# Products with v for halves of two neighbouring heads side by side, and one block-diagonal last product for both

## The reference

```python
B, H, S, D = 2, 8, 768, 64
mask = q_bucket[:, :, :, None] == k_bucket[:, :, None, :]
scores = np.where(mask, scale * q @ k.T, -1e9)
attn = np.exp(scores - scores.max(-1)); attn /= attn.sum(-1) + 1e-09
x = attn @ v                    # then [B*S, H*D]
logits = x @ w_gate             # 8 experts; the largest takes the token
eom = sigmoid(x @ w_output_gate)
out[token] = gate_w * eom * expert(x)     # then the dense pair
```

## Time and profile before

| | |
|---|---|
| median of 3 runs | 790.98 us |
| profiled execution | 790.95 us, span 789.1 us |
| granted TensorE clock, mean | 0.998 |
| TensorE busy | 775.8 us (98%), 4359 records |
| VectorE, ScalarE, GpSimd busy | 451.7, 376.7, 340.1 us |
| attention stage | up to about 263 us |
| records of `times_v` | 66.8 us busy in bank_b, 372 records |
| records of `last` | 23.5 us busy, 192 records |

### The profile page before, as it was taken

How to read it: one execution, slowest core, us unless ns; L and a number is a source line. 1 busy time by engine, 2 the same in 40 slices (tenths; PEclk the granted TensorE clock), 3 DMA queues, 4 the chain that set the end, 5 groups by cost and what they waited for, 6 DMA issues and landing times.

```text
span 789.1 us, 12941 instructions
## 1 busy us (share of the span) xinstructions
PE 775.8 (98%) x4359; PEld 652.8 (83%) x4359; DVE 451.7 (57%) x798; ACT 376.7 (48%) x714; POOL 340.1 (43%) x336
## 2 busy tenths in 40 slices
PE   8999999999999999999999999999999999999997
PEld 5777887788778678888888888899899889989985
DVE  6777777878786764454444544669337316613720
ACT  6787788778887242234431340057227206503610
POOL 4244335565653389797777981134210010000000
PEclk9999999999999999999999999999999999999999
DMA  6122322221100187567555640530010010000000
GB/s 199 59 78 88 104 68 78 56 57 41 52 11 11 47 308 257 190 235 238 172 191 178 236 160 27 174 121 1 27 54 1 9 59 15 1 14 28 1 13 27
DMA packets 40942, 72.68 MB, mean 92 GB/s; under 512 B 17904, under 2 KB 24304, under 8 KB 40880
## 3 DMA queue, kind: packets, MB, share of 16 engines
q10 hardware_dynamic: 9456, 31.53, 12.0%
q1 hardware_dynamic: 27984, 29.04, 11.7%
q0 software_dynamic: 3440, 11.28, 4.3%
HBM read 60.56 MB, written 11.28 MB: 91 GB/s over the span
## 4 chain that ended last, share of the span: by engine, by line
PE 62%; issue 28%; DVE 4%; POOL 2%; ACT 1%; DMA 1%; POOLq 0%; ACTq 0%; DVEq 0%
PE pair_s L1382 13%; PE pair_t L1397 13%; PE bank_b L1241 8%; PE pair_u L1225 8%; PE pair_s L1214 4%; PE pair_t L1214 4%; PE bank_b L1254 2%; PE pair_u L1361 2%; PE bank_a L1192 2%; PE bank_a L1178 1%; POOL out L606 1%; PE pair_s L1434 1%; DVE g_lo L1157 1%; PE bank_a L1200 1%; POOL y_raw L600 1%
## 5 line engine op out<-in xcount | busy, mean ns | idle before, releaser
L448 POOL TENSOR_TENSOR w_part<-w_raw,w_part 128x1024 fp32r<-128x1024 f32 x80 | 190.1, 2407 | 57.1 <-ACT w_part L703 56.4
L703 ACT ACTIVATE w_part<-w_raw 128x1024 fp32r<-128x1024 f32 x72 | 73.8, 1055 | 133.5 <-PE pair_t L1397 101.4
L1484 PE MATMUL pair_t<-w_part,g_hi 128*128 128x512 f32 x384 | 118.9, 391 | 0.3 <-POOL w_part L448 0.3
L1382 PE MATMUL pair_s<-w_part,xs_t 128*128 x456 | 108.7, 394 | 0.3 <-DVE xs_t L1035 0.3
L1397 PE MATMUL pair_t<-w_part,hid_t 128*128 x456 | 109.0, 394 | 0.0
L606 POOL DMA_INDIRECT out<-o_sb,token x12 | 11.8, 987 | 208.4 <-DVE o_sb L1127 208.4
L1382 PEld LDWEIGHTS pair_s<-w_part,xs_t 128*128 128x128 f32 x456 | 84.2, 188 | 17.6 <-issue 0.8
L1397 PEld LDWEIGHTS pair_t<-w_part,hid_t 128*128 128x128 f32 x456 | 84.4, 188 | 16.9
L805 ACT ACTIVATE elu<-elu 128x384 f32<-128x384 f32 x64 | 33.6, 525 | 123.2 <-DVE elu L1147 123.1
L1484 PEld LDWEIGHTS pair_t<-w_part,g_hi 128*128 128x128 f32 x384 | 71.6, 188 | 15.1 <-issue 0.7
L1225 PE MATMUL pair_u<-first,exps 128*128 128x128 f32 x564 | 78.5, 274 | 0.5 <-ACT exps_t L672 0.3
(11 more groups left out here) (220 smaller groups left out, 1249.7 us busy)
## 6 DMA issues: line engine op xcount, KB each, us to landing
w_raw<-in_moe_w ACTq DMA_DIRECT2D x48, 512.0 KB, 6.0
w_raw<-in_moe_w SPq DMA_DIRECT2D x16, 512.0 KB, 5.6
ys_sorted<-ys SPq DMA_DIRECT2D x19, 256.5 KB, 3.9
w_raw<-in_moe_w_in ACTq DMA_DIRECT2D x8, 512.0 KB, 5.9
raw<-in_q SPq DMA_DIRECT2D x16, 192.0 KB, 2.9
raw<-in_k SPq DMA_DIRECT2D x16, 192.0 KB, 2.8
v_nat<-in_v SPq DMA_DIRECT2D x16, 192.0 KB, 2.4
x_rows<-rows_sb SPq DMA_DIRECT2D x16, 192.0 KB, 2.3
```

What stands on the lines that cost most here:

```text
L448: pool.tensor_tensor(chunk_of(w_part, n, 1, c), w_raw[n % 2][c][:, :], chunk_of(w_part, n, 0, c).bitcast(F32), ALU.subtract).then_inc(s_wl ...
L703: act.activation(chunk_of(w_part, n, 0, c), w_raw[n % 2][c][:, :], ACT.Copy).then_inc(s_whi, 1)
L1382: mm = pe.matmul(pair_s[:, h, :], xs_t[:, xp, c * P:(c + 1) * P], w_part[:, bass.ds(par, 1), wp, a:a + 512], start=c == 0 and xp == 0 and ...
L1484: mm = pe.matmul(pair_t[:, t % 2, :], gp[:, f, j * P:(j + 1) * P], w_out_p[:, wp, f, :], start=f == 0 and m == 0, stop=f == FT - 1 and m == 2)
```

## The change

Work is cut into 17 units (`UNITS`) instead of 16 heads. The query tiles of a head are now taken in the order 3, 4, 5, 0, 1, 2 (`place_of`), and unit `u` holds the last three tiles taken of head `u - 1` and the first three of head `u`. Unit 0 has head 0 alone, unit 16 head 15 alone.

- `times_v(u)` has twelve products of 384 columns as before, all into one bank: v of head `u - 1` into partitions 0 to 63, v of head `u` into 64 to 127. Each pair runs over all six key tiles, so nothing is left to add. It is split over parts 0 and 1 as before, with no wait between. Units 0 and 16 (`times_v_alone`) have six products in the old way, even and odd key tiles apart. Unit 0 has its six in part 0; unit 16 has them behind the twelve of unit 15 in the last part 1.
- One `copy_u` a unit, in part 1.
- `last(u)` has three products of 160 columns: `last_w` is block-diagonal, [128, head, 2, 80], with the identity and the gates of one head for the upper partitions and of the other for the lower. `last_alone` has three of 80 with `last_e`.
- `exps_t` has room for four halves instead of two, so its copies wait for older products. v of a head is freed a unit later.
- `rows_of`, `copy_rows`, `inverse`, `store_rows` go by units; a store is two DMAs. `rows_of` always multiplies and adds; `logit` is zeroed first.
- At the start VectorE has three more memsets; ten gate DMAs instead of four go out behind the loads of head 2; GpSimd writes the identities of `last_e` in head 1 and those of `last_w` (two copies) in head 2.
- At the end both unit 15 and unit 16 go by the shorter way.

The diff, without the lines that only rename:

```diff
             rows_sb = sb("rows_sb", [P, 2, J, QE])
             u_sb = sb("u_sb", [P, S])
-            last_w = sb("last_w", [P, H, QE])
+            last_w = sb("last_w", [P, H, 2, QE])
+            last_e = sb("last_e", [P, 2, QE])
             raw = sb("raw", [P, 2, 2, J, D])
             q_a = sb("q_a", [P, 2, S], F32R)
...
-        u_bank = lambda g, h: bank_a if g == HEADS - 1 and h == 1 else bank_b
+        u_bank = lambda u: bank_a if u == HEADS else bank_b
+
+
+        place_of = lambda m: (m // J, (m % J + JH) % J)
+        unit_of = lambda m: (m + JH) // J
+        parts_of = lambda u: slice(JH if u == 0 else 0, JH if u == HEADS else J)
+
+        def turned_half(hh, part=slice(0, J)):
+            return exps_t[:, part, (hh % 4) * HALF:(hh % 4 + 1) * HALF]
+
+        def turned_tile(m, part):
+            a = (m // JH % 4) * HALF + m % JH * P
+            return exps_t[:, part, a:a + P]
 
         def cc(name, rows=P):
...
         @block.sync
         def _(sp):
 
-            def store_rows(g):
-                b, h = g // H, g % H
-                sp.wait_ge(s_x, g + 1)
-                sp.dma_start(x_dram.rearrange("(b j p) d -> b p j d", b=B, j=J)[b, :, :, h * D:(h + 1) * D],
-                             rows_sb[:, g % 2, :, 0:D]).then_inc(s_xst[g % 2], 16)
+            def store_rows(u):
+                sp.wait_ge(s_x, u + 1)
+                for g, at in ((u - 1, slice(0, JH)), (u, slice(JH, J))):
+                    if 0 <= g < HEADS:
+                        b, h = g // H, g % H
+                        sp.dma_start(x_dram.rearrange("(b j p) d -> b p j d", b=B, j=J)[b, :, at, h * D:(h + 1) * D],
+                                     rows_sb[:, u % 2, at, 0:D]).then_inc(s_xst[u % 2], 16)
 
...
-                    sp.wait_ge(s_av, 2 * (g - 3))
+                    sp.wait_ge(s_av, g - 2)
                 if g >= 2:
...
             load_v(1)
-            for r in range(2):
-                half = slice(r * D, (r + 1) * D)
+            def load_gates():
+                low, high = slice(0, D), slice(D, P)
                 for part, src in enumerate((w_gate, w_ogate)):
-                    a = D + part * E
-                    sp.dma_start(last_w[half, :, a:a + E], src.rearrange("(h d) e -> d h e", d=D)).then_inc(s_wg, 16)
+                    to = slice(D + part * E, D + (part + 1) * E)
+                    w = src.rearrange("(h d) e -> d h e", d=D)
+                    sp.dma_start(last_e[low, :, to], w[:, 0::H - 1, :]).then_inc(s_wg, 16)
+                    sp.dma_start(last_e[high, :, to], w[:, 0::H - 1, :]).then_inc(s_wg, 16)
+                    sp.dma_start(last_w[low, 1:H, 0, to], w[:, 0:H - 1, :]).then_inc(s_wg, 16)
+                    sp.dma_start(last_w[low, 0:1, 0, to], w[:, H - 1:H, :]).then_inc(s_wg, 16)
+                    sp.dma_start(last_w[high, :, 1, to], w).then_inc(s_wg, 16)
+
             for g in range(2, HEADS):
                 load_head(g)
+                if g == 2:
+                    load_gates()
                 if 3 <= g < 3 + NCH:
                     sp.dma_start(chunk_dst(0, g - 3), chunk_source(0, g - 3)).then_inc(s_wld[g - 3], 16)
-            for g in range(HEADS - 5, HEADS):
-                store_rows(g)
+            for u in range(HEADS - 5, UNITS):
+                store_rows(u)
             for i in range(2):
...
-                if h > 0:
-                    pool.wait_ge(s_sh, shares(g - 1) + 1)
-                    pool.tensor_tensor(to, to, part, ALU.add).then_inc(s_sh, 1)
-                pool.tensor_tensor(rows_sb[:, g % 2, :, 0:D], rows_sb[:, g % 2, :, 0:D], wide(D),
+            def rows_of(u):
+                pool.wait_ge(s_fr, u + 1)
+                pool.wait_ge(s_inv, u + 1)
+                if u == 0:
+                    pool.wait_ge(s_zero, 5)
+                at = parts_of(u)
+                wide = lambda n: den[:, u % 4, at].unsqueeze(2).broadcast_to([P, at.stop - at.start, n])
+                part = rows_sb[:, u % 2, at, D:QE]
+                pool.tensor_tensor(part, part, wide(2 * E), ALU.mult).then_inc(s_sh, 1)
+                pool.wait_ge(s_sh, shares(u - 1) + 1)
+                if u == H:
+                    to = logit[:, :, :].rearrange("p (q i) e -> p q i e", i=JH)[:, 0::3]
+                    part = part.rearrange("p (q i) e -> p q i e", i=JH)
+                else:
+                    to = logit[:, u // H * J + at.start:u // H * J + at.stop, :]
+                pool.tensor_tensor(to, to, part, ALU.add).then_inc(s_sh, 1)
+                pool.tensor_tensor(rows_sb[:, u % 2, at, 0:D], rows_sb[:, u % 2, at, 0:D], wide(D),
                                    ALU.mult).then_inc(s_x, 1)
...
-                    pool.tensor_copy(last_w[:, :, 0:D],
-                                     cc("twice").unsqueeze(1).broadcast_to([P, H, D])).then_inc(s_twice, 1)
+                    pool.tensor_copy(last_e[:, :, 0:D],
+                                     cc("twice").unsqueeze(1).broadcast_to([P, 2, D])).then_inc(s_twice, 1)
                     pool.wait_ge(s_twice, 1)
+                if g == 2:
+                    pool.wait_ge(s_cp, copies(5))
+                    for o in range(2):
+                        of = slice(o * D, (o + 1) * D)
+                        pool.tensor_copy(last_w[of, :, o, 0:D],
+                                         cc("twice")[of].unsqueeze(1).broadcast_to([D, H, D])).then_inc(s_twice, 1)
+                        pool.wait_ge(s_twice, 2 + o)
                 if g >= 9:
...
-            def copy_u(g, h):
...
+            def copy_u(u):
+                act.wait_ge(s_av, u + 1)
+                if u >= 2:
+                    act.wait_ge(s_fin, u - 1)
+                act.activation(u_sb[:, u % 2 * HALF:(u % 2 + 1) * HALF], u_bank(u)[:, 0:HALF], ACT.Copy).then_inc(s_u, 1)
+
+            def free_rows(u):
+                if u >= 2:
+                    act.wait_ge(s_x, u - 1)
+                    act.wait_ge(s_sh, shares(u - 2))
+                    act.wait_ge(s_xst[u % 2], 16 * (u - 1))
+
+            def copy_rows(u):
+                act.wait_ge(s_fin, u + 1)
+                free_rows(u)
+                turned_u = bank_b[:, 0:J * QE].rearrange("p (i o n) -> p o i n", i=JH, o=2)
+                to = rows_sb[:, u % 2, :, :].rearrange("p (o i) n -> p o i n", i=JH)
+                if u == 0:
+                    act.activation(to[:, 1], turned_u[:, 1], ACT.Copy).then_inc(s_fr, 1)
+                else:
+                    act.activation(to, turned_u, ACT.Copy).then_inc(s_fr, 1)
...
+                act.wait_ge(s_x, u)
+                for i in range(JH):
+                    for o in range(1 if u == HEADS else 2):
+                        qt = o * JH + i
+                        at = i * QE if u == HEADS else (2 * i + o) * QE
+                        bank = pair_t[:, 0, :] if u == HEADS else bank_b
+                        done = act.activation(rows_sb[:, u % 2, qt, 0:D], bank[:, at:at + D], ACT.Copy,
+                                              scale=den[:, u % 4, qt:qt + 1])
                 done.then_inc(s_x, 1)
 
...
-                if g >= 2 and part <= 1:
-                    copy_u(g - 2, part)
+                if g >= 2 and part == 1:
+                    copy_u(g - 2)
                 if g < HEADS and part == 1:
                     keep_low(g, 1)
                 if g < HEADS and part == 0:
                     mask_odd(g, 0)
                 if g + 1 < HEADS and part == 2:
                     split_hi(g + 1, 0)
+            copy_u(HEADS)
             last_rows(HEADS - 1)
+            last_rows(HEADS)
 
 
...
             dve.memset(proj_w[:, :, :].bitcast(F32), 0.0).then_inc(s_zero, 1)
+            dve.memset(last_w[0:D, :, 1, :], 0.0).then_inc(s_zero, 1)
+            dve.memset(last_w[D:P, :, 0, :], 0.0).then_inc(s_zero, 1)
+            dve.memset(logit[:, :, :], 0.0).then_inc(s_zero, 1)
 
...
+            inverse(HEADS)
             then(dve.memset(onehot[:, TILES, :], 0.0))
-            dve.wait_ge(s_inv, HEADS)
+            dve.wait_ge(s_inv, UNITS)
             dve.wait_ge(s_sh, shares(HEADS - 2))
             dve.wait_ge(s_fin, HEADS)
-            dve.tensor_tensor(lg_part[:, :, :], bank_b[:, 0:J * QE].rearrange("p (j n) -> p j n", n=QE)[:, :, D:QE],
-                              den[:, (HEADS - 1) % 4, :].unsqueeze(2).broadcast_to([P, J, 2 * E]),
-                              ALU.mult).then_inc(s_lg, 1)
+            dve.tensor_tensor(lg_part[:, :, :].rearrange("p (o i) e -> p o i e", i=JH),
+                              bank_b[:, 0:J * QE].rearrange("p (i o n) -> p o i n", i=JH, o=2)[:, :, :, D:QE],
+                              den[:, (HEADS - 1) % 4, :].rearrange("p (o i) -> p o i", i=JH).unsqueeze(3).broadcast_to(
+                                  [P, 2, JH, 2 * E]), ALU.mult).then_inc(s_lg, 1)
             dve.wait_ge(s_lg, 1)
             then(dve.tensor_tensor(logit[:, J:TILES, :], logit[:, J:TILES, :], lg_part[:, :, :], ALU.add))
+            dve.wait_ge(s_fin, UNITS)
```

(109 more changed lines are left out.)

58 lines of the change are left out of this document (21 added, 37 removed).

## The result

| | before | after |
|---|---|---|
| median, device us | 791.04 (12 runs, 790.78 to 791.72) | 792.71 (12 runs, 792.34 to 793.13) |
| profiled execution, span | 790.95, 789.1 | 792.53, 790.7 |
| TensorE busy in the span | 775.8 (98%) | 770.2 (97%) |

The ratio is 1.0019, with an interval of 1.0011 to 1.0027: slower by 0.19%, just inside the 0.2% that a measurement can tell from none, and 0.1 us from the forecast of 792.6. TensorE does 5.6 us less, and the kernel takes 1.7 us more.

What follows compares the result with a forecast made beforehand. The prediction took a ScalarE and VectorE chain plus TensorE's stretch from release to projection to set each head's period. 790.95 + 0.0 (heads) - 0.1 (start) + 1.8 (end) = 792.65, forecast 792.6 us; range 790.9 to 793.6.

Steps and rivals of the forecast that it cites:

- VectorE's copy is late next: Third part of each head: transposes still wait for `copy_t1(m_e)`, so the 0.48 us freed per unit counts nothing.
- The record of 160 columns: In `last`: each record takes 0.137 us with its weight load hidden, six take 0.82 instead of 1.30.
- The slack of TensorE before: Transposes in `turn_exps(m_e + 1)`, kernel before: TensorE could be only about 0.02 us early against VectorE's copy.
- the steady stage: Repeating heads of the attention stage: period stays 15.7 us, total effect 0.0.
- drift: VectorE's chain in the heads: 0.01 us an operation, seven operations, 13 heads, 0.9 us either way at most.
- Start: Head 2: six products before `project(2, 1)` go, but ScalarE's queue holds `keep_low` to 32.24 from 32.34, gain 0.1.
- head 2 gives back more: Rival: ScalarE's queue at head 2 moves up with the missing product, up to 1.3 us gained, 791.4; chance 0.10.
- The end: Last units of attention: moved products lie on the path, so routing and everything after start 1.8 us later.
- the start of the products: Final products with v, after `copy_rows(14)`: start at 256.70 instead of 256.96, a gain of 0.26 us.
- `last(15)` to VectorE: Attention's end: `last(15)` takes 0.85 us, `last_alone(16)` ends at 264.37, VectorE starts 0.14 behind, at 264.51.
- TensorE-bound: Rival: TensorE limits the heads after all, so 0.48 us comes off each of 13 heads, 785.2 us; chance 0.12.
- The load that isn't hidden: Rival: weight load of 160-column records in `last` stays exposed, 0.245 us a record, 795.1 us; chance 0.06.

Runs made afterwards that it cites:

- after_pad2: Changed kernel with two of the three 160-column products of `last` run twice in units 1 to 13: 792.56 us, period 15.70.
- after_short_copy: Changed kernel with part 2's `copy_t1(m_e)` cut to one of three blocks in groups 4 to 15: 789.65 us, period 15.450.
- before_short_copy: Kernel before with part 2's `copy_t1(m_e)` cut to one of three blocks in groups 4 to 15: 788.91 us, period 15.606.
- before_end_twice: Kernel before with the last six products with v (head 15, second half) run twice: 793.16 us, ratio 1.0027.
- after_copy_first: Changed kernel with VectorE's `copy_t1(m_e)` in part 2 ahead of `row_max(m_s + 1)`: 795.08 us, period 15.84.
- before_copy_first: Kernel before with VectorE's `copy_t1(m_e)` in part 2 ahead of `row_max(m_s + 1)`: 793.2 us, period 15.85.
- after_mask_last: Changed kernel with VectorE's `mask_even(g, 1)` moved behind `copy_t1(m_e)`: 801.03 us, period 16.25.
- before_mask_last: Kernel before with VectorE's `mask_even(g, 1)` moved behind `copy_t1(m_e)`: 797.94 us, period 16.27.
- before_pad: Kernel before with two of the six products of `last` run twice in heads 1 to 13: 795.24 us, period 16.053.

## Why the prediction was right

*The step on which it rests, VectorE's copy is late next, held.* The wait is 0.53 us in heads 1 to 12, but for one of 0.64 (head 13: 0.80), about 0.5 was forecast; the period stayed at 15.70. The added products of after_pad2 and the shorter copy of after_short_copy show this, the trace alone would only suggest it. TensorE's busy share of 103 to 240 us is 98%, as forecast.

*The record of 160 columns* takes 0.135 to 0.136, 0.137 was forecast from the streaming. Six of them take 0.82, as forecast. The Trainium skill ("TensorE: Matmul & The Clock Gate", section "The mechanism") says that a load overlaps running products only where its row group differs. By the prediction's rows that would make a record 0.245; by these 0.136 the load is not exposed. The same section also lets a load into a background weight buffer run ahead, and no run here tells which way the hardware takes.

*The slack of TensorE before was mis-sized*: 0.02 us in the text, 0.11 by the two periods of before_short_copy and before. My 0.02 counted the wait in front of the fourth transpose. After a wait the next transpose follows at 0.164 to 0.166 instead of 0.109, 0.055 more (in the kernel before 162.791 to 162.957 in head 8); the remaining 0.03 is unexplained. Here this changed nothing, as the freed time is wasted whatever the slack. It would have misjudged a change that *adds* work: 13 heads x 0.11 = 1.4 us are free, not 0.3. The same step should have given the steady stage a small gain instead of 0.0: once the wait is certain, TensorE's side no longer touches the period, and it fell by 0.014 a head, 0.18 in all. That lies within the bound of 0.9 which the text gave for drift.

*Start.* A gain of 0.1 was forecast, `keep_low(2)` at 32.24; it came at 31.95. Of the 0.39, 0.26 was there already when the first product's weights had landed:

```profile
5.55 0.16 DVE L942 CAST proj_w<-proj 64x6 fp32r<-64x6 f32 x1 [2.11 <-DMA proj<-in_proj]
...
29.42 0.55 DVE L892 SCALAR_TENSOR_TENSOR x_lo<-bank_a,k_b 128x384 fp32r<-128x384 f32 x1
...
30.03 0.44 PE L1252 MATMUL bank_a<-k_b,proj_w 128*128 128x384 f32 x1 [0.70 <-DVE x_lo L892]
...
31.43 0.49 ACT L715 ACTIVATE u_sb<-bank_b 128x384 f32<-128x384 f32 x1
31.95 0.49 ACT L690 ACTIVATE low_sb<-bank_a 64x384 f32<-64x384 f32 x1
```

5.55 against 5.81 is a transfer, which the change doesn't touch. The other 0.13 is the forecast's. The mechanism is as written: TensorE's projection now waits for `x_lo` and comes 1.6 us earlier, yet `keep_low` stands behind `copy_u` in ScalarE's queue. But this place lay anywhere from 31.86 to 32.90 in the executions looked at, of both kernels, so 0.1 can't be measured there, and the rival "head 2 gives back more" is refuted by its cause (`keep_low` does stand behind `copy_u`, and no 1.3 us come off anywhere), not by the time. The three memsets and the gate DMAs cost nothing that shows: VectorE still waits 2.11 us for that transfer where it waited 4.14. Of the difference of 2.03 the earlier transfer is 0.26, which leaves 1.77 for the memsets, 1.8 forecast.

*The end.* +1.89 from `keep_low(15)` to the last product with the gates, +1.82 forecast. Its terms: six products 1.92 (1.94 forecast); the start of the products 0.15 earlier instead of 0.26 (20.15 us behind `keep_low(15)`, against 20.30), because they start 0.15 behind the end of ScalarE's copy (255.50 + 0.59) and not 0.06; `last(15)` to VectorE 1.82 instead of 1.70, as forecast by 0.85 + 0.85 + 0.14 = 1.84. The one term that was off is the start of the products, by 0.1. VectorE's last product with the gates comes at 264.01, near 264.4 was forecast; the 0.4 are the earlier start of the whole. The stretch behind it, +0.3, of which the forecast had none, is no work of the change as far as the traces show: over the profiled executions of the seven kernels built on the one before it is 526.4 to 526.7 (one of 525.6), with 526.7 in before_end_twice, and over the six built on the one after 526.6 to 526.7. The two executions compared happen to lie near the two ends of this spread.

*The rivals.* TensorE-bound (785.2) is refuted by after_pad2. The load that isn't hidden (795.1) is refuted by the record. In sum: -0.4 - 0.2 + 1.9 + 0.3 measured, 0.0 - 0.1 + 1.8 forecast. The two terms that carry the forecast, the heads and the end, are right by their mechanism. That the total came within 0.1 us is in part luck: against the forecast stand -0.3 at the start, -0.2 in the heads, +0.1 at the end and +0.3 behind it, and they cancel.

*Where I was wrong* is in the expectations of the two reorderings, in both kernels: after_copy_first (-6.5 expected, +2.4 against after's own 792.71), before_copy_first, after_mask_last (-5.1 expected, +8.3) and before_mask_last. They took one edge of a tight engine and forgot who else waits on the same queue. before_pad was off by the slack (3.9 instead of 5.1). What the copy's place gives one consumer it takes from another, since VectorE is the chain.

## What to carry to other kernels

A TensorE that is busy 98 to 100% of a stage can still be early: look for a product group in the middle of which another engine's copy ends just when it is needed, and follow that engine back until it finds a gap. Adding the same small work to the kernel before and after is the cheapest test of which side binds, and shortening the suspected operation gives the other side's own period. Work pushed behind the last repetition of a pipelined loop was paid in full here, while what the change saved inside the loop was worth next to nothing: cost the drain first.

## What the runs showed of the hardware

- An fp32 product with a full 128 x 128 stationary block and 160 moving columns takes 0.136 us a record at 2.4 GHz, against 0.111 with 80 columns: twice the columns cost a quarter more. At the prediction's 0.84 ns a column 80 columns would stream in 0.067, so the streaming does not set the smaller one. That the load of the 128 x 128 block does is argued; no run changed the load alone.
- A transpose behind a wait is followed by the next at 0.164 instead of 0.109 us (the three at 162.26 span 0.55, undisturbed ones 0.49): a wait costs 0.055 us beyond itself. Where modelled ends hide the wait, they hide this too: in the kernel before TensorE is busy in all 137.00 us.
- Two kernels whose TensorE work differs by 0.48 us a head had periods 0.01 to 0.02 us apart, wherever a copy or mask of VectorE came late for TensorE (15.72 and 15.70, 15.85 and 15.84, 16.27 and 16.25).
